# Layer 1's second product in tiles of 384 tokens, and a reordered start, in a fused attention and two-layer feed-forward kernel

## What is computed

```python
kv  = einsum('bhsd,bhse->bhde', k, v)      # batch 4, heads 8, seq 576, head_dim 64
out = einsum('bhsd,bhde->bhse', q, kv)
x   = out / sqrt(mean(out**2, -1) + 1e-6) * g_norm      # then (2304 tokens, 512)
h   = x @ w_in                             # layer 1: 512 -> 2048
x   = (h * sigmoid(h)) @ w_out             #          2048 -> 512
x   = ((x @ w_a) * (x @ w_b)) @ w_out2     # layer 2: 512 -> 1536 -> 512
```

## Time and profile before

| | us |
|---|---|
| median of 3 runs (lowest, highest) | 881.95 (881.38, 883.39) |
| the profiled execution's own time | 881.7 |
| its span, first to last instruction | 879.9 |
| PE busy in it | 867.1 |
| DVE busy | 515.5 |
| POOL busy | 610.5 |
| ACT busy | 278.7 |

### The profile page before, as it was taken

One profiled execution on the slowest core, in us unless ns is written; L12 is line 12 of the kernel. 1 busy time (PEld: TensorE's weight loads), 2 busy tenths in 40 slices (PEclk: granted clock), 3 DMA queues, 4 the chain that ended last, 5 costly groups with the idle time before them and its releaser, 6 DMA issues.

```text
span 879.9 us, 17064 instructions
## 1 busy us (share of the span) xinstructions
PE 867.1 (99%) x6632; PEld 824.9 (94%) x6632; DVE 515.5 (59%) x817; ACT 278.7 (32%) x467; POOL 610.5 (69%) x889
## 2 busy tenths in 40 slices
PE   7999999999999999999999999999999999999998
PEld 6799999999999999999999999999999999999997
DVE  2666656657886666565775355464574553644536
ACT  2765434434443232222432121121152211212210
POOL 1575545666568787766668697887989876877760
PEclk9999999999999999999999999999999999999999
DMA  9864224111011111111101021011110340210103
GB/s 264 190 132 113 65 54 77 49 48 50 25 48 49 31 43 50 49 49 49 49 25 49 25 72 50 24 49 49 48 49 26 117 111 25 72 44 30 48 26 107
DMA packets 47263, 55.62 MB, mean 63 GB/s; under 512 B 11985, under 2 KB 32721, under 8 KB 47185
## 3 DMA queue, kind: packets, MB, share of 16 engines
q1 hardware_dynamic: 44384, 49.55, 20.8%
q10 hardware_dynamic: 2800, 4.98, 1.9%
HBM read 49.81 MB, written 4.72 MB: 62 GB/s over the span
## 4 chain that ended last, share of the span: by engine, by line
PE 95%; DMA 1%; DVE 1%; issue 1%; POOL 1%; SPq 1%; ACT 0%; DVEq 0%; POOLq 0%
PE ps L753 48%; PE ps L823 8%; PE ps L824 7%; PE ps L825 7%; PE ps L845 6%; PE ps L847 6%; PE ps L846 6%; PE ps L770 3%; PE ps L713 2%; DMA kvq<-in_q_dram 1%; PE ps L723 1%; PE ps L687 1%; PE ps L701 1%; DVE x_lo L1355 1%; SPq L457 0%
## 5 line engine op out<-in xcount | busy, mean ns | idle before, releaser
L753 PE MATMUL ps<-x_hi,w_hi 128*128 128x288 f32 x1064 | 229.2, 297 | 0.7 <-issue 0.3
L753 PE MATMUL ps<-x_lo,w_hi 128*128 128x288 f32 x1064 | 228.0, 296 | 0.0
L753 PE MATMUL ps<-x_hi,w_lo 128*128 128x288 f32 x1064 | 226.9, 295 | 0.0
L753 PEld LDWEIGHTS ps<-x_hi,w_hi 128*128 128x128 f32 x1064 | 175.1, 188 | 11.2 <-issue 2.6
L753 PEld LDWEIGHTS ps<-x_hi,w_lo 128*128 128x128 f32 x1064 | 171.7, 189 | 0.0
L753 PEld LDWEIGHTS ps<-x_lo,w_hi 128*128 128x128 f32 x1064 | 170.3, 188 | 0.0
L1095 ACT COPY kept<-ps 128x576 f32<-128x576 f32 x114 | 73.2, 642 | 295.6 <-PE ps L753 295.1
L823 PE MATMUL ps<-g_hi,d_hi 128*128 128x288 f32 x512 | 153.7, 300 | 2.2 <-DVE xy L1418 1.3
L504 POOL TENSOR_SCALAR w_hi<-wt 128x256 fp32r<-128x256 f32 x152 | 68.5, 451 | 119.1 <-PE ps L753 112.4
L1418 DVE TENSOR_TENSOR xy<-xy,ps 128x288 f32<-128x288 f32 x224 | 101.1, 453 | 85.5 <-PE ps L825 84.0
L825 PE MATMUL ps<-g_hi,d_lo 128*128 128x288 f32 x512 | 150.9, 295 | 0.0
(11 more groups left out here) (109 smaller groups left out, 1207.0 us busy)
## 6 DMA issues: line engine op xcount, KB each, us to landing
raw<-in_moe_w_out_dram SPq DMA_DIRECT2D x28, 512.0 KB, 3.7
raw<-in_moe_w_in_dram SPq DMA_DIRECT2D x15, 512.0 KB, 3.5
raw<-in_moe_w_a_dram SPq DMA_DIRECT2D x12, 512.0 KB, 3.6
raw<-in_moe_w_b_dram SPq DMA_DIRECT2D x12, 512.0 KB, 3.6
kvq<-in_k_dram SPq DMA_DIRECT2D x12, 288.0 KB, 13.9
kvq<-in_v_dram SPq DMA_DIRECT2D x12, 288.0 KB, 15.0
out_dram<-xy SPq DMA_DIRECT2D x26, 128.0 KB, 2.5
kvq<-in_q_dram SPq DMA_DIRECT2D x16, 144.0 KB, 6.3
```

The lines of the kernel that those rows point to most:

```text
L753: mm = pe.matmul(ps[:, bank + s, 0:PART], w, x[:, n, c, s * PART:(s + 1) * PART], start=(begins and first), stop=last, skip_group_check=no ...
```

## The change

1. Layer 1's second product has 12 tiles of 384 tokens by 128 outputs in place of 16 of 288. A pair's 1152 tokens are cut in thirds. The middle third reaches over both halves of `g`; in the 5 pairs of 16 where the two halves are not neighbours in the ring of three, it is read, and flushed, as two pieces of 192. Thirds 1 and 2 wait until both halves are ready.
2. The lists of tiles follow: after a pair's steps (2, 2, 2, 2, 2, 1, 1), after pair 1's plain steps (1, 2, 1, 2, ...), after the 14 steps of the first pair of layer 2 one each but none after steps 10 and 13. DVE's flushes are moved likewise, `next_rest(pp, 2)` goes behind `add(u, 0)`, two flushes and `silu(pp, 0)`, and in `second_pair` `last_sum` goes ahead of every flush.
3. In the head DVE takes over two of the four copies of the first kv. The normalised result of head pair 0 is made and turned before, or between, the copies and turns of head pair 1; for head pairs 1 and 2 DVE normalises before it copies.
4. The last head pair's q_kv goes to banks 6, 7, 3, so that the first half of `plain(1)` can run before the last `o_turn`s; `plain(2)` goes ahead of `attend(0)`.

```diff
-    D_TILES = {1: 4 * KT, 2: TOK_TILES}
+    CUT = SEQ - TILE3
+    D_TILES = {1: GTOK // TILE3 * KT, 2: TOK_TILES}
-    TILES_AFTER = (2, 3, 3, 2, 2, 2, 2)
+    TILES_AFTER = (2, 2, 2, 2, 2, 1, 1)
-    PLAIN_TILES_AFTER = 2
+    PLAIN_TILES_AFTER = (1, 2, 1, 2, 1, 2, 1, 2)
+    LAST_TILES_AFTER = (1, 1, 1, 1, 1, 1, 1, 1, 1, 1, 0, 1, 1, 0)
+    LAST_PRODS, LAST_TURNS = (6, 7, 3), (2, 6, 7)
...
+            def third_of(g, pp, third, f):
+                first, second = (2 * pp) % G_HALVES * SEQ, (2 * pp + 1) % G_HALVES * SEQ
+                if third == 0:
+                    return g[:, f, first:first + TILE3]
+                if third == 2:
+                    return g[:, f, second + CUT:second + SEQ]
+                if not crossed(pp):
+                    return g[:, f, first + TILE3:second + CUT]
+                pieces = g[:, f, 0:G_HALVES * SEQ].rearrange("p (n c) -> p n c", c=CUT)
+                return pieces[:, 0:G_HALVES * SEQ // CUT:G_HALVES * SEQ // CUT - 1, :]
...
@@ PE, head
             for h in range(PAIRS):
                 for j in range(JS):
-                    if h:
-                        o_turn(0, h - 1, j, first_bank(h - 1, j))
-                    q_kv(0, h, j, first_bank(h, j))
+                    if h > 1:
+                        o_turn(0, h - 1, j, result_bank(h - 1, j))
+                    q_kv(0, h, j, prod_bank(h, j))
                 if h + 1 < PAIRS:
                     kv(0, h + 1)
                     for j in range(JS):
+                        if h == 0:
+                            o_turn(0, 0, j, result_bank(0, j))
                         q_turn(0, h + 1, j, first_bank(h + 1, j))
             pe.wait_ge(x_kept, UNITS - JS)
             plain(0)
-            for j, bank in enumerate((2, 6, 7)):
-                o_turn(0, 3, j, bank)
-            pe.wait_ge(n_ready, UNITS)
-            plain(1)
+            pe.wait_ge(qT_kept, UNITS)
+            plain_half(0, 1, 0)
+            for j in range(JS):
+                o_turn(0, PAIRS - 1, j, result_bank(PAIRS - 1, j))
+            plain_half(0, 1, 1)
@@ DVE, second_pair
                 half_sum(1)
-                flush(0, 1)
+                last_sum()
+                flush(0, 0)
                 norm(at + 1)
-                flush(2, 3)
-                last_sum()
+                half_sum(2)
+                dve.wait_ge(*x_summed(0, 4))
+                flush(1, 2)
@@ DVE, layer1
-                next_rest(pp, 2)
                 add(u, 0, both(BANK_B))
-                flush(8, 9)
+                flush(6, 7)
                 silu(pp, 0)
+                next_rest(pp, 2)
...
                 add(u, 1, halves(held[:, 2, :]))
-                flush(12, 13)
+                flush(10, 10)
@@ DVE, head
+            second_kv_keep()
             for h in range(PAIRS):
                 for j in range(JS):
                     sums(0, h, j)
                 invert(0, h)
                 for j in range(JS):
-                    if h + 1 < PAIRS:
+                    normalise(0, h, j)
+                    if 0 < h < PAIRS - 1:
                         qT_keep(0, h + 1, j, first_bank(h + 1, j))
-                    normalise(0, h, j)
+                if h == 0:
+                    for j in range(JS):
+                        qT_keep(0, 1, j, first_bank(1, j))
```

More of the change, by code:

```diff
@@ L818, in down1 @@
                 wait_turn(bank)
-                part, cols = slice(at * SEQ + s * PART, at * SEQ + (s + 1) * PART), slice(d * P, (d + 1) * P)
-                dst = ps[:, bank, 0:PART]
+                cols = slice(d * P, (d + 1) * P)
+                dst = ps[:, bank, 0:TILE3]
+                if third == 1 and crossed(pp):
+                    dst = halves(dst)
                 for f in range(2):
                     hi, lo = d_hi[:, pp % 2, f, cols], d_lo[:, pp % 2, f, cols]
-                    pe.matmul(dst, hi, g_hi[:, f, part], start=(f == 0), stop=False)
-                    pe.matmul(dst, hi, g_lo[:, f, part], start=False, stop=False)
-                    mm = pe.matmul(dst, lo, g_hi[:, f, part], start=False, stop=(f == 1))
+                    of_high, of_low = third_of(g_hi, pp, third, f), third_of(g_lo, pp, third, f)
+                    pe.matmul(dst, hi, of_high, start=(f == 0), stop=False)
+                    pe.matmul(dst, hi, of_low, start=False, stop=False)
+                    mm = pe.matmul(dst, lo, of_high, start=False, stop=(f == 1))
                 mm.then_inc(down, 1)
@@ L894, in second_pair @@
                     plain_half(1, k, 1)
-                    for _ in range(PLAIN_TILES_AFTER):
+                    for _ in range(PLAIN_TILES_AFTER[k]):
                         down1(0, t)
@@ L1247, in _ @@
             half_round(6, 0)
-            for j, bank in enumerate((2, 6, 7)):
-                keep(0, 3, j, bank)
+            for j in range(JS):
+                keep(0, PAIRS - 1, j, result_bank(PAIRS - 1, j))
             first_pair()
@@ L1409, in flush1 @@
                 t = down0(pp) + n
-                m, d, s = down_order(n)
+                third, d = down_order(n)
                 G = SEGS[seg_of(pp)][0]
-                at = d * GTOK + m * SEQ + s * PART
-                dst, src = xy[:, G, at:at + PART], ps[:, tile_bank(t), 0:PART]
-                dve.wait_ge(down, t + 1)
-                if pp == PAIR0[seg_of(pp)]:
-                    nc.vector.tensor_copy(dst, src).then_inc(flushed, 1)
-                else:
-                    nc.vector.tensor_tensor(dst, dst, src, ALU.add).then_inc(flushed, 1)
+                at = d * GTOK + third * TILE3
+                dst, src = xy[:, G, at:at + TILE3], ps[:, tile_bank(t), 0:TILE3]
+                pieces = [(dst, src)]
+                if third == 1 and crossed(pp):
+                    pieces = [(dst[:, 0:CUT], src[:, CUT:]), (dst[:, CUT:], src[:, 0:CUT])]
+                dve.wait_ge(down, t + 1)
+                for dst, src in pieces:
+                    if pp == PAIR0[seg_of(pp)]:
+                        op = nc.vector.tensor_copy(dst, src)
+                    else:
+                        op = nc.vector.tensor_tensor(dst, dst, src, ALU.add)
+                op.then_inc(flushed, 1)
             def flush2(pp, j):
@@ L1510, in layer1 @@
                 attend(at + 1)
[L1511 removed]
+                flush(2, 3)
                 late_rest(pp, 4)
@@ L1526, in layer1 @@
                 attend(at + 3)
+                add(u, 0, both(BANK_B))
+                flush(6, 7)
+                silu(pp, 0)
                 next_rest(pp, 2)
-                add(u, 0, both(BANK_B))
-                flush(8, 9)
-                silu(pp, 0)
                 norm(at + 4)
@@ L1533, in layer1 @@
                 g_rest(pp, 0)
-                flush(10, 11)
+                flush(8, 9)
                 silu(pp, 1)
@@ L1616, in layer2, with second_kv_keep @@
                 next_rest(pp, 3)
+            def second_kv_keep():
+                dve.wait_ge(kv_mm, 1)
+                for odd in range(2):
+                    rows = slice(odd * HALF, odd * HALF + HD)
+                    cp = nc.vector.tensor_copy(kv_sb[rows, 0, 1, rows], ps[rows, BANK_D + 1, 0:HD])
+                cp.then_inc(kv_kept2, 1)
             for j in range(JS):
                 qT_keep(0, 0, j, first_bank(0, j))
+            second_kv_keep()
             for h in range(PAIRS):
```

81 lines of the change are left out of this document (45 added, 36 removed).

## The result

The changed kernel took 876.56 us (median of 4, 876.43 to 877.59), the kernel before 881.66 (median of 4): ratio 0.9941, 95% interval 0.9924 to 0.9958. The sign and the range were right (870.8 to 878.0), the forecast of 872.9 was 3.7 too low. The profiled execution of the changed kernel is its longest, 877.59 with a span of 875.8 and a mean clock of 0.996; the other three had 0.998.

The account below looks back on a forecast made before the run. PE was taken to bound the kernel, busy 867.1 of 879.9 us. 881.7 - 6.2 + 0.5 + 0.8 + 0.3 - 0.5 - 1.5 + 1.6 - 4.05 = 872.65, median 872.9 us; range 870.8 to 878.0.

Parts of the forecast that it names:

- Tiles of 384: Second product's tiles: 172.9 ns a matmul and no long first matmul in rows of three, -6.2 us together.
- rival (c): Tiles: 384 columns gain nothing in pace, 176.7 ns a matmul; +4.3, so 877.2 us; chance 5%.
- Attention, +0.3: Pairs with attention: normalise or sums also stand ahead of add(u, 1) at step 6; 0.3 us added.
- Crossed thirds, +0.5: In 5 pairs of 16 the middle third is read and flushed in two pieces; 0.5 us added.
- Step 6, +0.8: Layer 1 pairs: one tile before step 6 leaves 0.06 us waiting for add(u, 1), times 14, +0.8 us.
- Rival (b): Covers too short: DVE late by a further 0.3 us at step 6 in 14 pairs; 877.1 us; chance 14%.
- (e): Slower than before: add(u, 1) at step 6 stands behind tile 9's flush and silu(1); 889.4 us; chance 4%.
- Segment ends, -1.5: Ends of layer 1's segments: late first matmuls save 2.24 us, a later add(u, 1) costs 0.75; -1.5 us.
- `last_sum`, +1.6: Start of pair 1: last_sum ahead of flush 0 delays PE's kv, costing 1.6 us, bounds 0.8 and 2.5.
- The head, -4.05: Head: normalising and turning results earlier, plus half of plain(1) early, saves 4.05 us if the clock stays.
- rival (d): Head gives nothing back because PE's next instructions or data come no earlier; 876.9 us; chance 6%.
- rival (a): Head: the clock falls all the same, with 0.1 us holes in PE's work; +1.4, 874.3 us; chance 27%.

Follow-up runs that it names:

- experiment 8: experiment 3 with layer 1 tile lists (2, 2, 2, 2, 1, 2, 1) and tile 9's flush behind add(u, 1): 873.97 us, 0.9915.
- experiment 11: experiment 6 with next_rest(2) back ahead of add(u, 0), as before the change: 875.47 us, 0.9941.
- experiment 3: The changed kernel with last_sum behind the first flush and the normalise in pair 1: 875.45 us, 0.9937.
- experiment 2: The kernel before with the new head alone, tiles of 288 and lists as before: 882.35 us, 1.0016.
- experiment 5: The changed kernel with loads of head pairs 2 and 3 and the first weights held until the second head pair's q landed: 879.87 us, 0.9986.
- experiment 4: The changed kernel with loads of the last head pair and first weights held until the second head pair's q landed: 876.81 us, 0.9956.
- experiment 9: experiment 6 with head pair 0's three result turns together, ahead of head pair 1's three q_kv: 872.23 us, 0.9896.
- experiment 1: The changed kernel with the old head up to the first plain steps; tiles of 384, lists and last_sum stay changed: 875.39 us, 0.9941.
- experiment 6: experiment 3 with head pair 0's results turned between head pair 1's q_kv, not between the q turns; DVE still normalises first: 871.75 us, 0.9893.
- experiment 7: The changed kernel with 5 warming matmuls in place of 13 before the first kv: 878.88 us, 0.9968.
- experiment 10: experiment 6 with the tile lists of experiment 8: 871.19 us, 0.9884.

## Why the prediction was right in sign and 3.7 us off

- **Tiles of 384: right, mis-sized.** 174.2 ns for 172.9. A pair has 12 tiles of 6 matmuls, so 1.3 ns x 72 is 0.09 a pair. The usual pair went from 24.07 to 23.80, 0.27 where -0.41 and +0.06 were summed, 0.35; the 0.09 accounts for the missing 0.08. What step 6 costs beyond its 0.06 (below) is made good by the steps: without waits the seven take 11.14 (experiment 8), where I had put 11.20. The spacing of rival (c), 176.7, did not come.
- **Attention, +0.3: right.** Pairs 2 to 6 gained 0.95 where five usual ones gain 1.35; experiment 8 shows where, in pair 3 above all.
- **Crossed thirds, +0.5: wrong, nothing.** A crossed pair takes 23.79 or 23.81, as the others do, though 40 flushes of 192 columns stand in the trace.
- **Step 6, +0.8: right in kind, about half its size.** The wait is 0.06 by the rows, as forecast, but experiment 8 gives back 0.11 a pair, 1.5 us for 14. Rival (b), a further 0.3, did not occur, and (e) neither: DVE's add began in time.
- **Layer 2's first pair:** -0.92 where -0.5 and one batch of tiles, -0.27, were forecast.
- **Segment ends, -1.5: right, too small.** Pairs 7 and 15 lost 1.08 and 1.83; without the usual 0.27, 2.4 in all. What I had late next, `add(u, 1)`, was in time. At the first end the two low parts took 1.55 and 1.53 us apart, and 3.78 and 3.92 (experiment 11) back to back. Standing together is not what makes them long: at the second end, apart, one took 2.44 and the other 1.35. Each row of 2.44, in before, after and experiment 11, began while POOL was in a `d_lo` row (that of 429.82 in one that began at 429.75), and a `d_lo` row beside each took 2.4 us, where the median of POOL's 56 is 1.29. That agrees with the prediction's remark that POOL slows them; no run takes POOL's work away, so it stays a reading of the rows.
- **`last_sum`, +1.6: right.** 1.66 of idle; 1.47 by experiment 3.
- **All of these together** were forecast at -5.0 and came to -5.04. That it is so close is luck in part: in pairs 2 to 15 the usual gain was 3.8 us, where tiles, step 6 and crossed thirds had been summed to 4.4, and the segment ends gave back 0.9 more than forecast.
- **The head, -4.05: the step that failed.** The orders of DVE and PE did what I said up to 23.10, even 0.65 sooner than my 23.75. I then checked data ("the DMAs allow it"), but not PE's next instructions, though the row of 1.26 "issue" had made me list it as rival (d). The break of 3.03 us is that rival's, and behind it the clock sat at 0.50 for 6.8 us, as in rival (a), though by another road than its small holes. I had priced each alone, as a gain lost and as +1.4, and not that the one brings on the other. Together they took the 4.05 and 0.94 more, 4.99 in all. That is the whole miss of the profiled execution, whose span was forecast to shrink by 9.05 and shrank by 4.10; its time is 1.0 above the median. `plain(0)` at 41.46 is one of the signs that I had named for being wrong (later than 38), and 876.56 is within 0.4 of rival (d)'s 876.9, which I had given 6%. The other runs bear out the link: behind stops with 2.1 to 3.3 us of idle (experiments 2, 3, 5, 8) the clock fell to 0.50 as well, for 3.4 us or, in experiment 8, 6.8; behind those of 1.41 and 0.69 (4, 9) it did not.
- **The base.** The profiled execution of before lost its clock from 20.8 to 24.2, and I counted the return of those 1.4 us as gain. In experiment 1's set 11 of 15 executions of before had a mean clock of 1.00 and took 880.3 to 880.9. In experiment 6, whose head is without the break, pair 1 starts 3.38 before its place in the trace of before, close to the -4.05; but only 1.86 before that of experiment 1, whose old head kept its clock.

The numbers add up: +1.73 - 0.79 + 1.53 - 0.95 - 1.08 - 1.85 - 1.83 - 0.92 + 0.06 is -4.10, the difference of the spans. Experiment 6 is 3.7 us faster than experiment 3 (871.75 to 875.45; 0.9893 [0.9878, 0.9908] to 0.9937 [0.9925, 0.995]), by the order of the turns alone.

The Trainium skill's 2.5 ns beside columns ("TensorE: Matmul & The Clock Gate", section "Wait — 56ns, not 53.3ns?") would give 162.5 ns for 384 columns; the trace has 174.2, as it was 10 ns above that rule at 288. The line between two neighbouring rows was the better guide.

## What to carry to other kernels

A wait of PE that the trace calls "issue", at a fixed place in its stream, can be its instructions. It need not be: the 1.66 us of "issue" ahead of kv in pair 1 was a wait for DVE's flush. What told them apart was the row count and the packet's end. Before many short matmuls are packed closer together, as in a head, see when the instruction queue's next packet starts and how soon PE will have used up its block. And look in several executions whether the clock fell, before its return is booked as a gain.

## What the hardware did that I had not expected

- PE's instructions came in packets of 16 KB on a queue of their own, 256 rows each, and PE stopped where a block was used up and the next packet had not long been in. The 13 traces have 20 such stops: behind row 449 in all but experiment 7, behind row 705 in the changed kernel and experiments 2, 3, 4, 5, 8 and 9, behind row 961 in experiment 5. Each time PE went on 1.27 to 1.66 us behind the packet's end.
- When the packet for row 705 starts differs with the order of the work. With the old head it started at 22.27 and 22.29 (before, experiment 1), with experiments 6, 9, 10 and 11 at 22.65, 22.90, 22.93 and 22.94, with alternating turns at 24.39 (changed kernel), 24.81, 25.18, 24.20 (experiments 2, 3, 8), and with loads held back at 24.53 and 25.12 (experiments 4, 5). Counted from the end of the packet before it, that is 5.5 to 5.7 us without alternating turns and 7.4 to 8.5 with them.
- Experiment 7 doesn't fit a rule that goes by the order alone: its turns alternate, and its packet started at 23.56, 5.7 behind the one before. There PE ran at the lower clock and came to the turns only at 21.55. So what starts a packet, and why the alternating turns delay it by about 2 us, stays open. An early normalise does not do it (experiment 6), nor three q_kv in one piece (experiment 9).
